# The first phase's end in another order, its square copies on GpSimd, and level 0 ahead of the loop

## The reference

```python
for t in range(S):
    state = alpha[:, :, t, :, None] * state + np.einsum('bhd,bhe->bhde', k[:, :, t], v[:, :, t])
    y[:, :, t] = np.einsum('bhd,bhde->bhe', q[:, :, t], state)
# x is y with the heads side by side: (4, 768, 384)
xt = x.transpose(0, 2, 1)
u = x + (xt @ U @ V).transpose(0, 2, 1)
x = u + np.maximum(u @ w_ch1, 0.0) @ w_ch2             # 384 -> 1536 -> 384
h = np.maximum(x @ w_in, 0.0)                          # 384 -> 1024
u, v = h[..., :512], h[..., 512:]
v_n = (v - mean(v)) / sqrt(var(v) + 1e-6)              # over the last axis
out = (u * (einsum('ts,bsd->btd', w_spatial, v_n) + b_spatial[None, :, None])) @ w_out
```

## Time and profile before

| | us |
|---|---|
| median of 3 runs | 728.94 (727.58 to 729.64) |
| the profiled execution | 727.21, span 725.0 |
| PE busy | 696.3 (96%), 11336 products |
| PEld busy | 660.6 (91%) |
| DVE busy | 392.6 (54%) |
| ACT busy | 340.2 (47%) |
| POOL busy | 212.0 (29%) |

### The profile page before, as it was taken

One profiled execution on the slowest core, in us unless ns is written; L12 is line 12 of the kernel. 1 busy time (PEld: TensorE's weight loads), 2 busy tenths in 40 slices (PEclk: granted clock), 3 DMA queues, 4 the chain that ended last, 5 costly groups with the idle time before them and its releaser, 6 DMA issues.

```text
span 725.0 us, 25711 instructions
## 1 busy us (share of the span) xinstructions
PE 696.3 (96%) x11336; PEld 660.6 (91%) x11336; DVE 392.6 (54%) x666; ACT 340.2 (47%) x575; POOL 212.0 (29%) x143
## 2 busy tenths in 40 slices
PE   2689999999999999999999999999999999999998
PEld 2688989899899999999999999999998998999998
DVE  6888665545654654655453415125834852871671
ACT  5887654554654454556444332335532432532422
POOL 6704660410450320351220330461360060043022
PEclk9879999999999999999999999999999999999999
DMA  9415410410401221401100341011110101101001
GB/s 360 169 47 168 163 42 8 154 47 10 149 3 46 80 79 46 156 3 47 37 3 3 101 151 66 33 38 62 65 45 23 66 23 43 65 0 65 0 0 65
DMA packets 16524, 49.48 MB, mean 68 GB/s; under 512 B 1616, under 2 KB 9552, under 8 KB 15920
## 3 DMA queue, kind: packets, MB, share of 16 engines
q1 hardware_dynamic: 16432, 48.09, 18.8%
HBM read 38.65 MB, written 9.44 MB: 66 GB/s over the span
## 4 chain that ended last, share of the span: by engine, by line
PE 92%; ACT 3%; DVE 2%; issue 1%; DMA 1%; SPq 0%; DVEq 0%; ACTq 0%
PE HB L906 25%; PE ZB L994 7%; PE ZB L996 7%; PE ZB L995 7%; PE SB L906 6%; PE SB L782 5%; PE SB L1031 5%; PE ZB L906 4%; PE SB L888 2%; PE SB L1035 2%; PE ZB L1031 2%; PE ZB L1044 2%; PE SB L897 2%; PE SB L843 2%; PE SB L1044 2%
## 5 line engine op out<-in xcount | busy, mean ns | idle before, releaser
L1556 DVE SCALAR_TENSOR_TENSOR hid_lo<-HB,hid_hi 128x384 fp32r<-128x384 f32 x92 | 51.2, 556 | 139.7 <-ACT hid_hi L1238 139.3
L1238 ACT ACTIVATE hid_hi<-HB 128x384 fp32r<-128x384 f32 x92 | 45.3, 492 | 158.6 <-PE HB L906 158.5
L994 PE MATMUL ZB<-hid_hi,w2h 128*128 128x384 f32 x288 | 98.2, 341 | 0.0
L906 PE MATMUL HB<-uh,w1h 128*128 128x384 f32 x276 | 97.8, 354 | 0.2 <-DVE ul L1552 0.2
L996 PE MATMUL ZB<-hid_lo,w2h 128*128 128x384 f32 x288 | 96.5, 335 | 0.0
L995 PE MATMUL ZB<-hid_hi,w2l 128*128 128x384 f32 x288 | 96.3, 334 | 0.0
L906 PE MATMUL HB<-ul,w1h 128*128 128x384 f32 x276 | 92.5, 335 | 0.0
L906 PE MATMUL HB<-uh,w1l 128*128 128x384 f32 x276 | 92.4, 335 | 0.1
L1085 ACT COPY Qd<-Q 48x768 f32<-48x768 f32 x84 | 73.1, 871 | 12.8 <-POOL Q L674 4.3
L731 POOL TENSOR_TENSOR gl<-gf,gh 128x384 fp32r<-128x384 f32 x32 | 33.5, 1048 | 144.1 <-ACT gh L1278 143.8
L674 POOL TENSOR_TENSOR Q<-Q,bk 112x768 f32<-112x768 f32 x14 | 25.6, 1827 | 162.7 <-ACT Qd L1085 162.7
(11 more groups left out here) (269 smaller groups left out, 1516.5 us busy)
## 6 DMA issues: line engine op xcount, KB each, us to landing
Q<-in_q SPq DMA_DIRECT2D x8, 768.0 KB, 6.1
AL<-in_al SPq DMA_DIRECT2D x7, 768.0 KB, 4.5
K<-in_k SPq DMA_DIRECT2D x7, 768.0 KB, 4.2
Vt<-in_v SPq DMA_DIRECT2D x8, 576.0 KB, 3.6
mid<-x2s SPq DMA_DIRECT2D x8, 576.0 KB, 3.7
x<-mid SPq DMA_DIRECT2D x4, 1152.0 KB, 5.4
out<-o_sb SPq DMA_DIRECT2D x24, 192.0 KB, 1.8
x2s<-in_w SPq DMA_DIRECT2D x9, 384.0 KB, 5.1
```

The source lines that it names most:

```text
L906: last = nc.tensor.matmul(dst, weights(x, w), moving(y, m), start=(n == 0 and x == y == 0), stop=(n == total - 1 and y == 1))
L994: nc.tensor.matmul(bank, w2h[:, i, cols], hi, start=(i == 0), stop=False)
L1238: nc.scalar.activation(hid_hi[:, i % HID, :], up_bank(i)[:, 0:TILE], ACT.Relu).then_inc(h_hi, 1)
L1556: nc.vector.scalar_tensor_tensor(hid_lo[:, i % HID, :], up_bank(i)[:, 0:TILE], 0.0, hid_hi[:, i % HID, :].bitcast(F32), ALU.max, ALU.subtr ...
```

## The change

Four edits to the first phase:

- TensorE: level 0 of both groups is written out ahead of the loop, which now runs levels 1 to 5.
- GpSimd makes all eight square copies, after its last query scaling of the phase; it waits for the masked scores, for its own zeroing and for its own scaling. VectorE and ScalarE lose theirs.
- ScalarE walks the last steps in another order (`ACT_LAST`): group 1's key copies (step T) come ahead of its level-7 score copies. The first two weight casts keep their place behind both.
- The side space's third transpose bank is ZB[0] in place of ZB[2]: it is free once ScalarE has read the level-6 scores.

```diff
--- before.py
+++ after.py
@@ -218,9 +218,10 @@
 LEAD = [0.07] + [0.0] * (BATCH - 2)
 SLOTS = [step_slots(lead) for lead in LEAD]
 
+ACT_LAST = [(0, MASKED), (1, MASKED), (0, LEVELS - 1), (1, T_STEP), (1, LEVELS - 1)]
 LAST_STEPS = [(g, n) for n in range(MASKED, STEPS) for g in range(GROUPS)]
 
-HIGH1 = {(1, T_STEP): [0, 1], (0, KV_STEP): [2, 3], (0, Y_STEP - 1): [4], (1, Y_STEP - 1): [5]}
+HIGH1 = {(1, LEVELS - 1): [0, 1], (0, KV_STEP): [2, 3], (0, Y_STEP - 1): [4], (1, Y_STEP - 1): [5]}
 LOW1 = {(1, KV_STEP): [0, 1, 2, 3]}
 LAST_LOW1 = [4, 5]
 SPLIT_V = {(0, T_STEP): [0], (1, T_STEP): [1], (1, KV_STEP): [2]}
@@ -378,7 +379,7 @@
 
         main_space.SB, main_space.TB, main_space.KVB, main_space.YB = SB, SB, SB[0], [SB[1], SB[2], SB[0]]
         main_space.PB, side_space.PB = HB
-        side_space.SB, side_space.TB, side_space.KVB, side_space.YB = ZB, HB + ZB[2:], HB[1], ZB
+        side_space.SB, side_space.TB, side_space.KVB, side_space.YB = ZB, HB + ZB[:1], HB[1], ZB
 
 
         ld_q = [sem(f"ld_q{g}") for g in range(GROUPS)]
@@ -674,6 +675,15 @@
                 nc.gpsimd.tensor_tensor(qq, qq, t.broadcast_to([ROWS, FLAT // (2 * L), L]), ALU.mult
                                         ).then_inc(q_ready[g], 1)
 
+            def square_copies(g):
+                w = space(0, g)
+                pool.wait_ge(a_dve[g], taken(0, MASKED))
+                pool.wait_ge(zeroed_a[g], 1)
+                pool.wait_ge(q_ready[GROUPS - 1], MASKED - 1)
+                for r in QUARTERS:
+                    last = nc.gpsimd.tensor_copy(w.A[r, :, :, r], w.Ad[r, :, :, :])
+                last.then_inc(ad_copied[g], 2)
+
             def split(n):
 
                 where, loaded, value = slot(n)
@@ -742,6 +752,10 @@
             for n in range(2, MASKED):
                 for g in range(GROUPS):
                     scale_q(0, g, n)
+
+            for g in range(GROUPS):
+                square_copies(g)
+            pool.wait_ge(ad_copied[GROUPS - 1], 2)
 
             pool.wait_ge(w_lo, W1_PIECES - 2)
             pool.wait_ge(tot_ready[0], 2 * (LEVELS - 1))
@@ -1051,7 +1065,9 @@
                 last.then_inc(two_done, 1)
 
             pe.wait_ge(zeroed_s, 4)
-            with pe.Fori(0, MASKED) as n:
+            for g in range(GROUPS):
+                first_level(g, 0)
+            with pe.Fori(1, MASKED) as n:
                 for g in range(GROUPS):
                     first_level(g, n)
             for g, n in LAST_STEPS:
@@ -1310,9 +1326,7 @@
                     first_spread(g, n)
                     if n == 2:
                         pair_copy(g)
-            for g, n in LAST_STEPS:
-                if n == MASKED:
-                    square_copies(0, g, QUARTERS[:2])
+            for g, n in ACT_LAST + [s for s in LAST_STEPS if s not in ACT_LAST]:
                 att_step(0, g, n, True)
                 for m in HIGH1.get((g, n), []):
                     split_high(m)
@@ -1513,14 +1527,6 @@
                             last = nc.vector.scalar_tensor_tensor(w.Sc[:, p, c, :], w.Sc[:, p, c - 1, :], d, kv,
                                                                   ALU.mult, ALU.add)
                     last.then_inc(state_step[g], 1)
-
-            def square_copies(g, rows):
-                w = space(0, g)
-                dve.wait_ge(a_dve[g], taken(0, MASKED))
-                dve.wait_ge(zeroed_a[g], 1)
-                for r in rows:
-                    last = nc.vector.tensor_copy(w.A[r, :, :, r], w.Ad[r, :, :, :])
-                last.then_inc(ad_copied[g], 1)
 
             def split_v(part):
 
@@ -1695,9 +1701,6 @@
                     att_piece(0, g, n, piece, True)
                 if n == MASKED:
                     first_queries(g, n)
-                if (g, n) == (1, MASKED):
-                    for h in range(GROUPS):
-                        square_copies(h, QUARTERS[2:])
                 if (g, n) == (0, T_STEP):
                     key_copies(g)
                 if n == KV_STEP:
```

## The result

The changed kernel takes 746.58 us (median of 6 runs, 742.54 to 748.43) against 728.26 us before (6 runs, 726.65 to 729.64): ratio 1.0242, 95% interval 1.0208 to 1.0275. The profiled execution took 748.43 us with a span of 746.3, against 727.21 and 725.0. The forecast, 734.5 us, had the direction right and the size wrong: 18 us were lost where 5.8 were forecast, and the time lies outside 728 to 739. The profiled execution of the changed kernel is the slowest of its six, so a loss read from profiles is up to 3 us larger than one between medians. All times given as measured are medians of the fast executions; one of e11 (737.62 us), one of e12 (1717.55) and one of the kernel before beside them (774.91) were slow and are left out.

The account below looks back on a forecast made before the run. TensorE was taken to bound the kernel from 62 us on, bound by others until about 35 us. Pages +4.7, GpSimd clash +1.1 and clock 0 made +5.8 us: 733.0 profiled, 734.7 as median, stated as 734.5; range 728 to 739.

Parts of the forecast that it names:

- What bounds the kernel: From 62 us on TensorE is busy 656.23 of 663.00 us; the first phase's delay is carried to the end unaltered.
- The page term: Level 1, first phase: level 0 outside the loop makes TensorE stop for late code pages at 449 and 705; +4.7 us.
- The clash with GpSimd: Level 6, first phase: VectorE's four scalings each wait for one GpSimd copy's rest; +1.1 us, bounds +0.3 and +3.7.
- Square copies off VectorE: Around level 7: nothing gained, as the transposes wait for TensorE itself; worth 2.2 us were that cover gone.
- Order and bank: End of first phase: group 1's key copies earlier, weight casts some 2 us later; 0, at worst +0.5 us.
- Clock: After level 6, first phase: the same drop to half clock as before; 0, bounds -4 and +2 us.
- Page in time: Rival, level 1: the page packet comes before 17 us, leaving only the scalings' wait for GpSimd; 729.8 us, 14%.
- Faster by the clock: Rival: pages in time, level-6 hole gone, GpSimd's copies give way, clock stays 1.00 after 38.96 us; 725.7 us, 14%.
- VectorE starves: Rival, level 6: all GpSimd copies go ahead of VectorE's scalings, group 1's level 7 starts at 46.1 us; 737.3 us, 14%.
- The loop refetches: Rival, first-phase loop over three pages: each of five passes fetches at least twice; +15 us, 744 us, 3%.

Follow-up runs that it names:

- e11: Kernel before with 27 tiny products at TensorE's start and the later start-up loads held back until group 1's level 1 is scored; 730.74 us, ratio 1.0038.
- e12: e11 with 37 more tiny products at the start of the mixing layer, to put later page edges back; 733.34 us, ratio 1.0077.
- e5: Changed kernel with 31 tiny products (124 instructions) ahead of level 7, putting later page edges back where they lay before; 734.4 us, ratio 1.0082.
- e6: Kernel before with 33 tiny products (132 instructions) ahead of level 7, moving later page edges to where the changed kernel has them; 739.0 us, ratio 1.0152.
- e1: Changed kernel with TensorE's level 0 put back into the loop; 728.13 us, ratio 1.0007.
- e8: Changed kernel with GpSimd's three second-pass subtractions for the w2 low parts replaced by memsets to zero; 740.23 us, ratio 1.0159.
- e4: Kernel before with only ScalarE's new order of last steps and the side space's third transpose bank in ZB[0]; 728.76 us, ratio 1.0013.
- e3: Kernel before with only the eight square copies moved to GpSimd; 727.9 us, ratio 1.0001.
- e7: Changed kernel with SyncE issuing the later start-up loads only once group 1's level 1 is scored; 738.87 us, ratio 1.0147.

## Why the prediction was wrong, point by point

- *What bounds the kernel; carried "to the end of the kernel unaltered. The rest of the kernel holds no edited line that can wait long."* This is the step that failed. It costed 388 more instructions only where their pages are crossed in the first phase. They also move every later edge by 132 instructions of 256, and the prediction had the page size, the edges and a second-pass clash in its hands. In its place the runs show 15.3 us lost behind the first phase, of the profiled 21.3 (about 12 of 18.3 by medians). e5, with the edges back, loses 0.7 us there; e6, with the edges moved and nothing else, loses 8.1. e1 shows that nothing but the peel starts it. What a moved edge costs goes by what its late page sets off, and by when TensorE reaches it: with GpSimd's subtractions gone, e8 loses 4.5 us there.
- *The page term, +4.7.* Right in mechanism and place (27 and 57 products). First page: forecast 20.4 us, measured 20.23. Second: the spread came at 27.62, forecast 26.1, bounds 24.4 and 29.5. Level 6 of group 0 starts at 41.95 instead of 35.51: +6.4, so the term was 1.7 too small. The lag of the second packet was taken at 2.8 us and measured at 3.99 (20.23 to 24.22), which is 1.2 of it; the 0.2 us for three register instructions did not show. That the first page fits so well is in part luck: the lag was taken from one trace, and four other kernels of this series had it 4 us shorter. Those four all have level 0 in the loop, so none tells whether the break could have stayed away here.
- *The clash with GpSimd, +1.1.* Right in mechanism. A copy took 1.17 and 1.32 us, not the 0.82 taken from the cast, and level 7 of group 1 went from 42.38 to 49.41, +7.0: the clash added 0.6 to the 6.4. The Trainium skill's rule (SBUF — State Buffer, Practical consequences) fits these four scalings, each held up by one copy's rest at most; it does not fit the one of 5.98 us, which outwaited four of GpSimd's operations (97.61 to 102.80 us). What makes the difference was not tried.
- *Square copies off VectorE, 0.* Right here; and e12 shows the cover: where group 1's level 7 takes 1.56 us instead of 2.77 and ends at 43.89 instead of 45.15, the transposes wait 1.57 us for VectorE, which the prediction put at 2.2 us.
- *Order and bank, 0.* Right (e4: 1.0013, 0.9995 to 1.003).
- *Clock, 0, bounds -4 and +2.* In the first phase right: half clock in 47.0 to 53.8 us, for 38.96 to 49.20, while the way from group 1's level 7 to its first Y product got 1.0 us shorter (8.51 for 9.52). So +6.4, +0.6 and -1.0 make +6.0, where +4.7, +1.1 and 0 made the 5.8 forecast: the sum fits better than its terms, and that is luck. Outside it, two more such stretches came, each with a long stop of TensorE ahead of it or inside, and no bound held them.
- *The rivals.* Page in time: refuted by both breaks, though in e1, e3, e4 and e6 the packet did come at about 14 us, as this rival had it. Faster by the clock: refuted. VectorE starves: refuted at the copies (they take turns), but it is what happened at 97.63 us, in a place that the rival did not name. The loop refetches: refuted, one packet in four passes. The prediction's case against it misread one number: the loop of the gated layer has 324 products (756 instructions in the trace), not 282; that is still three pages. The two-block window that the Trainium skill (Runtime: NRT & Kernel Launch, Instruction fetch mechanics) gives would have had many.

What stays open: why the first packet of the start comes at about 14 or at about 18 us; why the page in e8 came 3.60 us after its predecessor's entry with the DMA idle (in e7 one came 5.6 us after, entered at 95.31 us, at a DMA share of 0.01); and 2.3 of the 15.3 us, which no step above holds. That the order of the load of AL and the page decides the break at 151 us is read from three traces; no run moved either alone.

## What to carry to other kernels

Where an engine runs long unrolled stretches of tiny instructions, code that is added counts modulo the page (here 256 instructions): move the edges on paper through the whole program, and look at every edge that falls into a stretch issued faster than a page comes, above all one beside a load. Such an edge is a risk and not a price: the same edge cost 1.80 us or nothing by half a microsecond. A few dummy instructions that put the later edges back tell in one run whether a loss comes from the change or from where its code lies. And a term carried "unaltered to the end" holds only if the other engines' meetings were checked at the new times.

## What the runs showed of the hardware

- TensorE's code comes page by page, with one packet between two breaks, and work went on 1.37 to 1.49 us after the late packet's end (four breaks of after). Counted from the entry of the predecessor, the packet's lag was 0.9 us with the DMA idle, 1.7 in e7 and 3.6 in e8, also idle; 3.95 us at 86.4% share; and 3.2 to 8.1 us in the start-up with the DMA full. So the entry of the predecessor is when a page is asked for at the earliest; the two long idle lags (3.6 in e8, 5.6 in e7) say that it can be later, or take longer.
- With later loads held back (DMA share 0.03 in 14 to 20 us of e7) the breaks of level 1 were 1.27 and 2.00 us, beside loads at full DMA share 3.26 and 4.46.
- A loop over three pages was not fetched again in four passes (one packet in 24.9 to 43.8 us of after).
- TensorE's granted clock was 0.52, which is the lower of its levels, 1.2 GHz, in 101.6 to 108.4 us, which begins inside the stop of 4.93 us (98.8 to 103.7), and in 152.8 to 159.6 us, with the stop of 1.80 us up to 153.64 in it; in the same stretches of the kernel before it was 1.00.
- A two-operand scaling on VectorE beside GpSimd took 1.47 to 1.57 us against copies of 1.2 to 1.3 us, and 3.16 to 5.98 us against GpSimd's own two-operand work of 1.0 to 1.8 us each, where 0.95 is its time alone.
